# A chain of a linear-attention stage, a gated feed-forward and eight experts: the feed-forward in tiles of 512 tokens, with its output projection turned round

## The reference

```python
# 1. attention with a decaying state: q, k, v, a of shape (4, 8, 768, 48)
#    its result is laid out as x: 3072 tokens x 384
# 2. gated feed-forward, d_model 384, d_ff 1536
a = x @ w_a                      # (3072, 1536)
b = x @ w_b
x2 = (a * b) @ w_out             # (3072, 384)
# 3. eight experts, 384 -> 1024 -> 384, one for each token
logits = x2 @ w_gate             # (3072, 8)
expert = argmax(logits)
gate = 1 / sum(exp(logits - max(logits)))
out[token] = gate * (relu(x2[token] @ w1[expert]) @ w2[expert])
```

## Time and profile before

| | |
|---|---|
| median of 3 runs | 1402.39 us |
| the profiled execution | 1407.39 us, its span 1405.1 us |
| TensorE busy | 1263.2 us, 90% |
| VectorE, ScalarE, GpSimd busy | 711.4, 655.4, 181.5 us |
| mean granted TensorE clock over the span | 0.958 |
| feed-forward, first product to last projection | 580.90 to 1089.08 us |

### The profile page before, as it was taken

One profiled execution on the slowest core, in us unless ns is written; L12 is line 12 of the kernel. 1 busy time (PEld: TensorE's weight loads), 2 busy tenths in 40 slices (PEclk: granted clock), 3 DMA queues, 4 the chain that ended last, 5 costly groups with the idle time before them and its releaser, 6 DMA issues.

```text
span 1405.1 us, 30441 instructions
## 1 busy us (share of the span) xinstructions
PE 1263.2 (90%) x12814; PEld 1187.2 (84%) x12814; DVE 711.4 (51%) x1085; ACT 655.4 (47%) x1225; POOL 181.5 (13%) x188
## 2 busy tenths in 40 slices
PE   2799999999999985599999999999999499999996
PEld 2688888888888875599999999999999399999996
DVE  2699999999999973511211212120213244444442
ACT  6688878878887722422222222222222144444442
POOL 1000000000000000021323132322224111111111
PEclk9699999999999995699999999999999699999998
DMA  6135445544556265400100010100001233333333
GB/s 112 35 106 140 131 120 147 172 126 122 142 130 186 88 206 175 146 16 2 35 1 34 1 34 1 35 6 13 17 1 63 62 126 126 132 130 127 127 132 109
DMA packets 198743, 126.93 MB, mean 90 GB/s; under 512 B 159436, under 2 KB 178675, under 8 KB 198624
## 3 DMA queue, kind: packets, MB, share of 16 engines
q1 hardware_dynamic: 194272, 115.72, 28.6%
q0 software_dynamic: 4352, 9.47, 1.9%
HBM read 73.04 MB, written 53.70 MB: 90 GB/s over the span
## 4 chain that ended last, share of the span: by engine, by line
PE 53%; POOL 2%; DVE 1%; issue 1%; DMA 1%; ACT 1%; POOLq 0%; ACTq 0%
PE m_a L1264 11%; PE m_b L1264 11%; PE e_y L1374 9%; PE e_h L1362 9%; PE m_x L1274 9%; DVE WL L1118 1%; POOL pl L1085 1%; POOL meta_scratch L1078 1%; PE e_tr L1348 1%; PE m_tr L1301 1%; DMA xe<-xs_scratch 1%; PE m_tr L1287 1%; PE m_tr L1295 1%; ACT ph L1009 0%; DMA xs_scratch<-x2s,pos 0%
## 5 line engine op out<-in xcount | busy, mean ns | idle before, releaser
L1188 DVE TENSOR_TENSOR pr<-asb,m_b 128x384 f32<-128x384 f32 x96 | 53.2, 554 | 374.9 <-ACT asb L1003 374.9
L702 PE MATMUL score<-QK 96*64 96x32 f32 x5376 | 186.3, 226 | 18.2 <-DVE QK L541 10.1
L702 PEld LDWEIGHTS score<-QK 96*64 96x64 f32 x5376 | 174.3, 141 | 30.9 <-DVE QK L541 14.9
L1003 ACT COPY asb<-m_a 128x384 f32<-128x384 f32 x96 | 46.1, 480 | 300.5 <-PE m_b L1264 300.5
L1085 POOL TENSOR_TENSOR pl<-pr,ph 128x384 fp32r<-128x384 f32 x96 | 96.3, 1004 | 381.2 <-ACT ph L1009 381.0
L541 DVE TENSOR_TENSOR QK<-QK,E 96x1536 f32<-96x1536 f32 x80 | 140.3, 1754 | 4.6 <-PE score L702 4.6
L1362 PE MATMUL e_h<-xeh,early 128*128 128x512 f32 x384 | 121.0, 393 | 1.6 <-DVE xel L1224 1.6
L1235 DVE SCALAR_TENSOR_TENSOR hl<-e_h,hh 128x512 fp32r<-128x512 f32 x64 | 44.2, 691 | 150.1 <-ACT hh L1041 150.1
L1274 PE MATMUL m_x<-WH,ph 128*128 128x384 f32 x288 | 99.4, 345 | 16.5 <-POOL pl L1085 16.5
L1274 PE MATMUL m_x<-WL,ph 128*128 128x384 f32 x288 | 97.1, 337 | 0.0
L1274 PE MATMUL m_x<-WH,pl 128*128 128x384 f32 x288 | 97.1, 337 | 0.0
(11 more groups left out here) (215 smaller groups left out, 3086.2 us busy)
## 6 DMA issues: line engine op xcount, KB each, us to landing
xs_scratch<-zeros SPq DMA_DIRECT2D x16, 2304.0 KB, 9.5
raw<-w SPq DMA_DIRECT2D x19, 1536.0 KB, 6.9
xe<-xs_scratch SPq DMA_DIRECT2D x9, 768.0 KB, 6.3
raw_re<-a_re SPq DMA_DIRECT2D x32, 144.0 KB, 2.9
raw_im<-a_im SPq DMA_DIRECT2D x32, 144.0 KB, 3.2
raw_k<-k SPq DMA_DIRECT2D x32, 144.0 KB, 3.0
raw_q<-q SPq DMA_DIRECT2D x32, 144.0 KB, 3.4
vB<-v SPq DMA_DIRECT2D x64, 72.0 KB, 2.9
```

The lines of the kernel that those rows point to most:

```text
L702: last = pe.matmul(score[n % 2][CH * g:CH * g + CH, a * HALF:(a + 1) * HALF], KT[i][0:R2, h, c * CH:(c + 1) * CH], x, start=True, stop=True)
L1003: act.copy(asb[:, f % 2, :], ap_[f % 2][:, 0:TW]).then_inc(s["a_out"], 1)
L1188: dve.tensor_tensor(pr[:, f % 2, :], asb[:, f % 2, :], bp_[f % 2][:, 0:TW], ALU.mult).then_inc(s["prod_done"], 1)
```

## The change

- `TT` becomes 4: 6 tiles of 512 tokens, 72 steps instead of 96. `ph` and `pl` become rings of three (512 wide).
- `project` is turned round: for each of the three groups d of 128 output columns, a 128x128 piece of w_out stands and 512 tokens of `ph` or `pl` move. The result has output columns on partitions.
- The loops over tiles and steps become one over n = 0 to 73 on TensorE: `project(n - 2)` follows `products(n)`, across the ends of tiles.
- ScalarE copies the result straight to `xt` at step 1 of the next tile (`columns_out`); the logits are made from it at step 3, all 12 in a row. The transpose back to rows, for the scatter alone, stands in steps 6 to 9 (`transpose_rows`, `rows_out`).
- `choose` stands at step 3, `ranks`, `place` and `gates` at step 5; the scatters of rows at 7 to 10, those of `meta` behind steps 6 and 11, two each. `X_STEPS` are 8, 9, 10.
- The three pieces of x of the first tile get a PSUM bank each.

```diff
-TT = 3
+TT = 4
-R_STEPS = (1, 2, 3)
-C_STEP = 5
-K_STEP = P_STEP = EXP_STEP = 6
-X_STEPS = (7, 8, 9)
+L_STEP = C_STEP = 3
+EXP_STEP = 4
+K_STEP = P_STEP = 5
+ROW_STEPS = (6, 7, 8, 9)
+X_STEPS = (8, 9, 10)
+S_STEPS = (7, 8, 9, 10)
-M_STEPS = {10: (0, 1), 11: (2,)}
+M_STEPS = {6: (0, 1), 11: (2, 3)}
...
-            ph = sbt(c1, "ph", [P, 4, TW], F32R)
-            pl = sbt(c1, "pl", [P, 4, TW], F32R)
+            ph = sbt(c1, "ph", [P, 3, TW], F32R)
+            pl = sbt(c1, "pl", [P, 3, TW], F32R)
...
# ScalarE
             for k in range(KD):
-                x_high(0, k)
+                x_high(0, k, TB[k])
...
+            def columns_out(T, d):
+                if d < KD - 1:
+                    act.wait_ge(s["x2_filled"], T * (KD - 1) + d + 1)
+                else:
+                    act.wait_ge(s["mm3_done"], T * NF + NF)
+                act.copy(xt[:, d, :], x2p[d][:, 0:TW]).then_inc(s["x2_out"], 1)
+            def rows_out(T, i):
+                bank = RB[i] if T == TILES - 1 else trp
+                act.wait_ge(s["rt_filled"], T * TT + i + 1)
+                if T and i == 0:
+                    act.wait_ge(s["scattered"], 16 * TT * T)
+                act.copy(x2s[:, i, :], bank[:, 0:DM]).then_inc(s["rt_out"], 1)
...
+                if n:
+                    m = n - 1
+                    if m > 2:
+                        act.wait_ge(s["mm3_done"], m - 2)
+                    act.wait_ge(s["prod_done"], m + 1)
+                    act.copy(ph[:, m % 3, :], pr[:, m % 2, :]).then_inc(s["ph_done"], 1)
...
# TensorE
+            def project(n):
+                T, f = divmod(n, NF)
                 pe.wait_ge(s["pl_done"], n + 1)
-                for t in range(TT):
-                    for i, (A, B) in enumerate(((ph, WH), (pl, WH), (ph, WL))):
-                        last = pe.matmul(x2p[t][:, 0:DM], A[:, f % 4, t * P:(t + 1) * P], wo_(B, f), start=(f == 0 and i == 0), stop=(f == NF - 1 and i == 2))
-                last.then_inc(s["mm3_done"], 1)
+                for d in range(KD):
+                    if T and f == 0:
+                        pe.wait_ge(s["x2_out"], (T - 1) * KD + d + 1)
+                    for i, (A, B) in enumerate(((ph, WH), (pl, WH), (ph, WL))):
+                        last = pe.matmul(x2p[d][:, 0:TW], wo_(B, f, d), A[:, n % 3, :], start=(f == 0 and i == 0), stop=(f == NF - 1 and i == 2))
+                    if f == NF - 1 and d < KD - 1:
+                        last.then_inc(s["x2_filled"], 1)
+                last.then_inc(s["mm3_done"], 1)
...
+            for n in range(STEPS + 2):
+                T, f = divmod(n, NF)
+                if n < STEPS:
+                    ...
+                    products(n)
+                    if T and f == L_STEP:
+                        logits(T - 1)
+                    if T and f == K_STEP:
+                        ranks(T - 1)
+                    if T and f in ROW_STEPS:
+                        ...
+                        transpose_rows(T - 1, i)
+                ...
+                if n >= 2:
+                    project(n - 2)
+                if T < TILES - 1 and f in X_STEPS:
+                    k = X_STEPS.index(f)
+                    ...
+                    if T and k < 2:
+                        pe.wait_ge(s["rt_out"], (T - 1) * TT + 3 + k)
+                    transpose_x(T + 1, k, trp)
+            pe.wait_ge(s["prod_done"], STEPS)
+            logits(TILES - 1)
             for i in range(TT):
-                transpose_x2(TILES - 1, i)
-            for i in range(TT):
-                logits(TILES - 1, i)
+                transpose_rows(TILES - 1, i)
             ranks(TILES - 1)
```

More of the change, by code:

```diff
@@ L883, in experts @@
         more = info[0:1, 2 * SLOTS:2 * SLOTS + 1]
[L885 to L891, removed]
         XB = [et[0], et[1], et[0]]
@@ new lines, in _ @@
+            for n in range(STEPS + 1):
+                T, f = divmod(n, NF)
+                if n < STEPS:
+                    if n > 1:
+                        act.wait_ge(s["prod_done"], n - 1)
+                    act.wait_ge(s["ab_filled"], n + 1)
+                    act.copy(asb[:, n % 2, :], ap_[n % 2][:, 0:TW]).then_inc(s["a_out"], 1)
+                if n:
[4 more added lines that the diff above has]
+                    act.copy(ph[:, m % 3, :], pr[:, m % 2, :]).then_inc(s["ph_done"], 1)
+                if n == STEPS:
+                    break
+                if T and f == 1:
+                    for d in range(KD):
+                        columns_out(T - 1, d)
+                if T and f == EXP_STEP:
+                    exponentials(T - 1)
+                if T and f in ROW_STEPS:
+                    rows_out(T - 1, ROW_STEPS.index(f))
+                if T < TILES - 1 and f in X_STEPS:
+                    x_high(T + 1, X_STEPS.index(f), trp)
+                if T == TILES - 1 and f in W_STEPS:
+                    k = W_STEPS.index(f)
+                    act.wait_ge(s["raw1_in"], 16)
+                    act.copy(w1h[:, k, :], raw1[:, k, :]).then_inc(s["w1_high"], 1)
@@ L1026, in _ @@
+            for d in range(KD):
+                columns_out(TILES - 1, d)
             for i in range(TT):
-                gate_x(TILES - 1, i)
+                rows_out(TILES - 1, i)
             exponentials(TILES - 1)
@@ L1277, in transpose_x @@
-            def transpose_x(T, k):
-                if k:
-                    pe.wait_ge(s["xl_done"], T * KD + k)
-                elif T > 1:
-                    pe.wait_ge(s["rank_out"], T - 1)
-                if k == 0:
-                    pe.wait_ge(s[f"xin_in{T % 2}"], 16 * (T // 2) + 16)
-                for t in range(TT):
-                    last = pe.transpose(trp[:, t * P:(t + 1) * P], xin[T % 2][:, t, k * P:(k + 1) * P], idn[:, :])
+                for d in range(KD):
+                    if T and f == 0:
[4 more added lines that the diff above has]
+                        last.then_inc(s["x2_filled"], 1)
@@ L1288, in transpose_x, with transpose_rows @@
+                last.then_inc(s["mm3_done"], 1)
+            def transpose_x(T, k, bank):
+                for t in range(TT):
+                    last = pe.transpose(bank[:, t * P:(t + 1) * P], xin[T % 2][:, t, k * P:(k + 1) * P], idn[:, :])
                 last.then_inc(s["tr_filled"], 1)
-            def transpose_x2(T, i):
-                bank = TB[i] if T == TILES - 1 else trp
-                pe.wait_ge(s["x2_out"], T * TT + i + 1)
+            def transpose_rows(T, i):
+                bank = RB[i] if T == TILES - 1 else trp
@@ L1294, in transpose_x2, with logits @@
                 for k in range(KD):
-                    last = pe.transpose(bank[:, k * P:(k + 1) * P], x2s[:, i, k * P:(k + 1) * P], idn[:, :])
+                    last = pe.transpose(bank[:, k * P:(k + 1) * P], xt[:, k, i * P:(i + 1) * P], idn[:, :])
                 last.then_inc(s["rt_filled"], 1)
-            def logits(T, i):
-                pe.wait_ge(s["rt_out"], T * TT + i + 1)
-                for k in range(KD):
-                    last = pe.matmul(logits_of(T)[:, i * NE:(i + 1) * NE], xt[:, i, k, :], wgs[:, k, :], start=(k == 0), stop=(k == KD - 1))
+            def logits(T):
+                pe.wait_ge(s["x2_out"], T * KD + KD)
+                for i in range(TT):
+                    for k in range(KD):
+                        last = pe.matmul(logits_of(T)[:, i * NE:(i + 1) * NE], xt[:, k, i * P:(i + 1) * P], wgs[:, k, :], start=(k == 0), stop=(k == KD - 1))
```

186 lines of the change are left out of this document (83 added, 103 removed).

## The result

The changed kernel took 1389.57 us (median of 4 runs, 1389.00 to 1390.05), beside 1402.59 for the kernel before: ratio 0.9905, 95% interval 0.9876 to 0.9934. The gain is 13.0 us, clear of the noise but under 1%, where 37.6 us were forecast; the time lies outside the range. One execution of the kernel before, in a later set, took 1816.14 us at a granted clock of 0.641 and is left out of every comparison.

A forecast was written before the change was run, and what follows sets the result against it. The prediction took TensorE's instruction stream to bound the feed-forward. Its terms, -13.3 - 20.5 - 2.3 - 2.5 + 1.0 = -37.6 us, brought the median from 1402.39 to 1364.8 us, range 1358 to 1377.

The forecast's parts named there:

- the cadence: Feed-forward matmuls on TensorE: 216 nines of 512 columns at 2.045 us replace 288 at 1.58, gaining 13.3 us.
- the inserts: Transposes, logits and ranks between a tile's matmuls: five sets of 5.44 us replace 29.5 us in all, gaining 2.3.
- rival (B): Feed-forward matmuls cost in proportion to their width, 234 ns at 512 columns, so no gain there: 1378.1 us, chance 6%.
- Drain: TensorE's waits for pl at tile ends: 7 of 8 go, 1.3 us left instead of 21.8, gaining 20.5.
- the last drain: The one wait for pl left at the very end of the feed-forward, put at 1.3 us.
- Start: Before the feed-forward's first product: high parts on ScalarE, subtractions on VectorE, first product at 578.4 instead of 580.90, gaining 2.5 us.
- Tail: From the last projection's end to the load of xe: 14.1 us instead of 13.1, a loss of 1.0.
- the slow start: The feed-forward's first two pieces run at half clock, 3.0 us, with the same half-clock stretch expected after the change.
- (C): New TensorE waits in routing steps 5 to 10, at bank m_tr, cost 12 us: 1376.8 us, chance 13%.
- (D): The low part pl comes late for its projection in every step, ending slower, say 45 us: 1410 us, chance 3%.
- (E): The waits at tile ends only move, to columns_out, costing 14 us: 1379 us, chance 3%.

## Why the prediction was wrong

Two steps failed, the cadence and the inserts.

*Cadence, forecast -13.3.* This step failed. It took the 227.2 ns of e_h for the new matmuls, "as its form is exactly the new one". Form and stage were compared, the place of the operands wasn't; the sign was there in the trace, as e_y stood at 174.6 and the same shape in the feed-forward at 175.6. Measured: nines of 2.08 to 2.12, 7.8 us lost in the stage, and the width worth 5.0 us in all. The gap formula of the Trainium skill (TensorE: Matmul & The Clock Gate, Back-to-back issue gap), which the page gives for an isolated matmul and which the prediction put beside rival (B) at 6%, made it an estimate of 1.7: as a gain that was nearer for this kernel, though its 215.8 ns at 512 columns were seen nowhere (227 at the best).

*Drain, forecast -20.5.* Right. 18.8 by itself in the kernel before, 19.1 worked out for seven; the last drain is 0.6 us of waiting, where 1.3 was forecast. pl took 1.285 us against 1.34 taken:

```profile
L1103 POOL TENSOR_TENSOR pl<-pr,ph 128x512 fp32r<-128x512 f32 x72 | 92.5, 1285 | 365.8 <-ACT ph L1025 365.8
```

*Inserts, forecast -2.3.* Failed, by about 9 us. The count of passes was right, and the working had no line for what 24 of them in a row do to the clock: four falls of 1.55 us, 6.2 in all. A further 2.9 us is price. The kernel with pieces of six and 128 bytes of shift shows it, as it has neither falls nor places that disagree: the logits of one tile start at 670.85 and those of the next at 750.49, so a tile lasts 79.64 us; less 36 x 2.045 = 73.62 there are 6.0 us of inserts, by the same working that gave 4.21 before, where 5.44 was put down. The working priced the passes that were added by themselves, while the nine behind them takes longer too:

```profile
673.59 0.57 PE m_tr L1315 x6
674.16 2.17 PE m_a L1283 x9
```

That is 0.13 us over the 2.04 of the others. As to the clock, the Trainium skill (TensorE: Matmul & The Clock Gate, Part 1: The HAM clock gate) says that a block on the chip sets it by how busy TensorE has been of late; the prediction has the lower level only at the start of the stage. The traces here show that it also falls where the profile has TensorE busy without a gap, behind 24 passes in 2.58 us; what that block counts, no run shows.

*Start, -2.5.* Right: -2.8. *Tail, +1.0.* Right in size: +1.4, and the load of xe 6.75 instead of 9.08, which its bounds did not have.

In sum: stage 473.2 forecast, 489.9 measured. Of the 16.7 between, 7.8 are place, 6.2 clock and 2.9 the inserts' price; the last drain gives back 0.7 and the slow start 0.3 (4.21 + 2.62 less 2 x 2.08 is 2.7, where 3.0 was put down); 0.8 is left over. Start, tail and experts cost nothing more: from the attention's end to the last instruction the two first profiles differ by 20.7 us where 37.6 were forecast, 16.9 less. The measured medians missed by 24.8; the other 8 us lie in the attention and in which executions were drawn, and the prediction had no term for a stage that varies by 10 us on its own.

*The range.* The bounds that it lists, 9 us up and 4 down, give 1361 to 1374 around 1364.8 and not 1358 to 1371, and the cadence's own lower bound, no gain at all, is 1378.1, outside the range of 1358 to 1377. The measured 1389.57 lies outside by either.

*The rivals.* (C), waits at the bank `m_tr`, did not happen: no wait of that kind within the stage. (D) and (E) neither. (B) had the right term, the cadence, and the wrong mechanism: steps of 234 ns do occur at 512 columns, but the same width takes 227 where the places agree. That the times of (E) and (B), 1379 and 1378.1, are nearer to the measured one than the forecast is luck as far as their mechanisms go.

## What to carry to other kernels

When a term is a rate taken from another place of the trace, compare the addresses of the operands too, not only the shape; a tile of unused bytes is the cheapest experiment there is. Narrow matmuls belong in small pieces between wide ones, however convenient one burst is: here six or twelve in a row never brought the clock down (20 and 10 places), and 24 did in most places. And take apart what an edit bundles: one loop across tiles, with 384 tokens, gave 18.8 us in this stage, as much as the whole change.

## What the runs showed of the hardware

- TensorE's matmul rate depends on where its operands start in SBUF relative to each other: 227 ns for 512 columns when all agree modulo 256 bytes, 230 to 235 on the average of nine when they don't; for 384 columns 173.7 against 174.6 to 175.6 (`e_y`: 14.59 us for 84, against 14.67 and 14.75). The Trainium skill (TensorE: Matmul & The Clock Gate, Part 2, Step-by-step) says that loading the next weights doesn't steal read bandwidth from the running matmul. Whether that holds here no run shows: they show some 2% (7.8 of 483.7 us) that depend on the two addresses, and not by what way.
- The granted clock can fall to its lower level for 3.4 us while TensorE has no idle time at all, behind 2.58 us of 8-column matmuls: behind four of five such bursts in the changed kernel, behind two of five with 128 bytes of shift. It costs 1.55 to 1.6 us.
- In the first 90 us the clock's way up differs between executions of the same program, and the end of the attention with it: 37 us at the lower level and 562.4 us in one profile of the changed kernel, 27 and 556.8 in the other; 553 to 564 us over all kernels.
